# One-core attention and expert kernel: the sinks' rows of v loaded once and split on GpSimd, buffers cleared by VectorE, the first weights' rounding moved

## What is computed

```python
def _attn_ref(q, k, v, n_sink, window):       # q, k, v: 2 x 8 x 768 x 64, n_sink 4, window 128
    scores = scale * np.matmul(q, k.transpose(0, 1, 3, 2))
    keep = is_sink | in_window                # the first 4 keys, and the last 128 up to the query
    scores = np.where(keep, scores, -1e9)
    a = np.exp(scores - np.max(scores, axis=-1, keepdims=True))
    a = a / (np.sum(a, axis=-1, keepdims=True) + 1e-09)
    return np.matmul(a, v)

x = attention, laid out as 1536 tokens x 512
x = layernorm(h * softmax(h)) * g_ln @ w_out       # h = x @ w_in, 512 -> 1024 -> 512
out = sum over 8 experts of P[:, e] * (relu(x @ w1[e]) @ w2[e])   # P: Sinkhorn gate of x @ w_gate
```

## Time and profile before

| | |
|---|---|
| median of 3 runs | 1252.02 us (1251.76 to 1252.05) |
| the profiled execution, its own time | 1253.09 us |
| its span, first to last instruction | 1251.3 us |
| TensorE's granted clock | 1.00 over the whole span |
| busy: PE, DVE, ACT, POOL | 99%, 55%, 29%, 43% |
| DMA engines busy, mean, slices of 31 us | 6, 4 and 4 tenths in the first three, then 0 to 1 |

### The profile page before, as it was taken

The page is one execution under the profiler, slowest core; times in us unless marked ns, Lnnn a source line. Parts: engine busy times, 40 slices in busy tenths (PEclk is TensorE's granted clock), DMA queues, the critical chain, the costliest instruction groups (busy, mean ns, idle before and its releaser), DMA issues.

```text
span 1251.3 us, 18785 instructions
## 1 busy us (share of the span) xinstructions
PE 1236.2 (99%) x6446; PEld 1097.3 (88%) x6446; DVE 691.7 (55%) x1348; ACT 365.1 (29%) x832; POOL 535.7 (43%) x625
## 2 busy tenths in 40 slices
PE   7999999999999999999999999999999999999998
PEld 4558899989988999999999999999999999999997
DVE  7895734356665555555555555555555555555554
ACT  7884634312233222222222222222222222222221
POOL 7772315644444444444444444444444444444440
PEclk9999999999999999999999999999999999999999
DMA  6440000111110111111111111111111111111102
GB/s 204 156 149 18 1 1 1 34 35 34 34 35 28 38 36 36 34 34 34 34 34 34 34 34 34 34 34 34 34 34 34 34 34 34 34 34 34 35 18 101
DMA packets 57264, 53.13 MB, mean 42 GB/s; under 512 B 4352, under 2 KB 44544, under 8 KB 57216
## 3 DMA queue, kind: packets, MB, share of 16 engines
q1 hardware_dynamic: 56928, 52.19, 13.1%
q10 hardware_dynamic: 288, 0.33, 0.1%
HBM read 49.35 MB, written 3.15 MB: 42 GB/s over the span
## 4 chain that ended last, share of the span: by engine, by line
PE 95%; ACT 2%; DVE 2%; DMA 1%; issue 1%; SPq 0%; DVEq 0%; ACTq 0%
PE ps L797 30%; PE ps L798 30%; PE ps L799 30%; PE ps L722 2%; PE ps L766 1%; PE ps L742 1%; PE ps L847 1%; ACT probs L1042 1%; ACT acc L1218 1%; DVE probs L1270 1%; DMA k_sb<-kT 0%; PE ps L977 0%; DVE xw L1303 0%; ACT xw L1066 0%; DMA q_sb<-qT 0%
## 5 line engine op out<-in xcount | busy, mean ns | idle before, releaser
L1528 DVE SCALAR_TENSOR_TENSOR acc<-ps,gate_now,acc 128x512 f32<-128x512 f32 x336 | 252.1, 750 | 166.2 <-PE ps L799 162.0
L797 PE MATMUL ps<-ring 128*128 128x512 f32 x768 | 300.6, 391 | 0.0
L798 PE MATMUL ps<-ring 128*128 128x512 f32 x768 | 299.8, 390 | 0.0
L799 PE MATMUL ps<-ring 128*128 128x512 f32 x768 | 299.2, 390 | 0.0
L1200 ACT ACTIVATE sums<-ps 128x384 f32<-128x384 f32 x192 | 94.4, 492 | 597.8 <-PE ps L799 597.8
L1504 DVE TENSOR_TENSOR sums<-ps,sums 128x384 f32<-128x384 f32 x192 | 106.9, 557 | 158.2 <-ACT sums L1200 106.9
L799 PEld LDWEIGHTS ps<-ring 128*128 128x128 f32 x768 | 144.3, 188 | 30.9
L797 PEld LDWEIGHTS ps<-ring 128*128 128x128 f32 x768 | 144.2, 188 | 27.9 <-DVE acc L1524 0.4
L798 PEld LDWEIGHTS ps<-ring 128*128 128x128 f32 x768 | 144.2, 188 | 25.8
L642 POOL TENSOR_TENSOR w_raw<-w_raw 128x256 f32<-128x256 f32 x32 | 23.7, 741 | 321.3 <-PE ps L799 321.3
L797 PE MATMUL ps<-xw,ring 128*128 128x384 f32 x448 | 152.5, 340 | 0.3 <-ACT sums L1200 0.2
(11 more groups left out here) (148 smaller groups left out, 1765.2 us busy)
## 6 DMA issues: line engine op xcount, KB each, us to landing
w_in<-w_exp SPq DMA_DIRECT2D x64, 256.0 KB, 3.2
w_raw<-w_exp SPq DMA_DIRECT2D x64, 128.0 KB, 2.8
w_raw<-w_exp SPq DMA_DIRECT2D x32, 256.0 KB, 3.2
v_sb<-v SPq DMA_DIRECT2D x16, 192.0 KB
out<-acc SPq DMA_DIRECT2D x12, 256.0 KB, 2.0
q_sb<-qT SPq DMA_DIRECT2D x7, 384.0 KB, 4.4
k_sb<-kT SPq DMA_DIRECT2D x7, 384.0 KB, 4.9
k_sb<-kT SPq DMA_DIRECT2D x9, 256.0 KB, 5.7
```

The lines of the kernel that those rows point to most:

```text
L797: pe.matmul(o, ws[0], xs[0], start=first, stop=False, skip_group_check=True)
L798: pe.matmul(o, ws[0], xs[1], start=False, stop=False, skip_group_check=True)
L799: return pe.matmul(o, ws[1], xs[0], start=False, stop=last, skip_group_check=True)
L1528: dve.scalar_tensor_tensor(out=acc[:, T, :], in0=y_bank(u, T), scalar=gate_now[:, T:T + 1], in1=acc[:, T, :], op0=ALU.mult, op1=ALU.add).t ...
```

## The change

The sinks' rows of v get a tile for all 8 pairs (`[72, 8, 128]` in place of `[72, 2, 128]`) and are loaded once, by six DMAs, which stand behind the first segment in SP's queue. POOL rounds them and takes the rest, for two pairs at a time, behind pairs 0, 2, 4 and 6 (`split_v_sinks`); `rest_v_sinks` on DVE is gone. The memsets of `v_sink`, `sink_cols`, `wg` and `ones` go from POOL to DVE, ahead of its first work. In pair 0 POOL rounds segment 0 between `normalise` 0 and `normalise` 1, takes the rest of `w_in` behind `lay_sinks`, and the rest of `w_out` behind `split_sinks`.

```diff
-        v_sink = sb("v_sink", [SINK_ROWS, 2, P], F32, in_a)
-        v_sink_r = sb("v_sink_r", [SINK_ROWS, 2, P], F32R, in_a)
+        v_sink = sb("v_sink", [SINK_ROWS, PAIRS, P], F32, in_a)
+        v_sink_r = sb("v_sink_r", [SINK_ROWS, PAIRS, P], F32R, in_a)
...
             def load_v(p, h):
                 sp.dma_start(v_sb[:, p % 2, h, :], v[p, h]).then_inc(v_loaded[p % 2], 16)
+
+            def load_v_sinks(h):
                 for row in (0, 32, 64):
                     row += h * NS
-                    sp.dma_start(v_sink[row:row + NS, p % 2, h * DH:(h + 1) * DH],
-                                 v[p, h, 0:NS, 0:DH]).then_inc(v_loaded[p % 2], 16)
+                    sp.dma_start(v_sink[row:row + NS, :, h * DH:(h + 1) * DH],
+                                 v[:, h, 0:NS, 0:DH].rearrange("p n d -> n p d")).then_inc(v_sinks_loaded, 16)
...
-            sp.wait_ge(consts, 2)
             for h in range(2):
                 load_v(0, h)
             load_segments(0)
+            sp.wait_ge(v_sinks_clear, 1)
+            for h in range(2):
+                load_v_sinks(h)
...
-            pool.memset(v_sink[:, :], 0.0).then_inc(consts, 1)
...
-            pool.memset(sink_cols[:, :, :].bitcast(F32), 0.0).then_inc(sinks_hi, 1)
...
-            pool.memset(ones[:, :], 1.0).then_inc(consts, 1)
-            pool.memset(wg[:, :, :].bitcast(F32), 0.0).then_inc(consts, 1)
...
+            def split_v_sinks(p):
+
+                two = slice(p, p + 2)
                 if p == 0:
-                    pool.wait_ge(consts, 2)
-                pool.tensor_scalar(v_sink_r[:, p % 2, :], v_sink[:, p % 2, :], 1.0, 0.0,
+                    pool.wait_ge(v_sinks_loaded, 96)
+                pool.tensor_scalar(v_sink_r[:, two, :], v_sink[:, two, :], 1.0, 0.0,
                                    ALU.mult, ALU.add).then_inc(v_sinks_hi, 1)
+                pool.wait_ge(v_sinks_hi, p // 2 + 1)
+                low = v_sink_r[64:SINK_ROWS, two, :]
+                pool.tensor_tensor(low, v_sink[64:SINK_ROWS, two, :], low.bitcast(F32),
+                                   ALU.subtract).then_inc(v_sinks_split, 1)
+                pool.wait_ge(v_sinks_split, p // 2 + 1)
...
             for p in range(PAIRS):
                 normalise(p, 0)
-                if p > 0:
+                if p == 0:
+                    round_segments(0)
+                else:
                     rest_w_in(p)
                 normalise(p, 1)
                 if p + 1 < PAIRS:
                     lay_sinks(p + 1)
                 if p == 0:
-                    round_segments(0)
                     rest_w_in(0)
-                rest_w_out(p)
+                else:
+                    rest_w_out(p)
                 if p == 4:
                     rest_router()
                 normalise(p, 2)
                 split_sinks(p)
-                round_v_sinks(p)
+                if p == 0:
+                    rest_w_out(0)
+                if p % 2 == 0:
+                    split_v_sinks(p)
                 if p + 1 < PAIRS:
                     round_segments(p + 1)
...
-                if t == 3 and p > 0:
-                    rest_v_sinks(p - 1)
...
+            dve.memset(v_sink[:, :, :], 0.0).then_inc(v_sinks_clear, 1)
+            dve.memset(sink_cols[:, :, :].bitcast(F32), 0.0).then_inc(sink_cols_clear, 1)
+            dve.memset(wg[:, :, :].bitcast(F32), 0.0).then_inc(router_clear, 1)
+            dve.memset(ones[:, :], 1.0).then_inc(ones_set, 1)
             dve.memset(top[:, 3:4], -0.5).then_inc(exponent, 1)
```

More of the change, by code:

```diff
@@ L219, in solu_moe @@
         sinks_hi, sinks_split = sem("sinks_hi"), sem("sinks_split")
+        sink_cols_clear, router_clear, ones_set = sem("sink_cols_clear"), sem("router_clear"), sem("ones_set")
+        v_sinks_clear, v_sinks_loaded = sem("v_sinks_clear"), sem("v_sinks_loaded")
         v_sinks_hi, v_sinks_split = sem("v_sinks_hi"), sem("v_sinks_split")
@@ L503, in _ @@
             pool.memset(mask1[:, 0:NS], 0.0).then_inc(masks, 1)
-            pool.memset(sink_cols[:, :, :].bitcast(F32), 0.0).then_inc(sinks_hi, 1)
-            pool.wait_ge(consts, 2)
+            pool.wait_ge(consts, 1)
             pool.affine_select(out=ident[:, :], in_=ident[:, :], compare_op=ALU.not_equal, fill=1.0,
                                base=0, pattern=[[-1, P]], channel_multiplier=1).then_inc(consts, 1)
-            pool.memset(ones[:, :], 1.0).then_inc(consts, 1)
-            pool.memset(wg[:, :, :].bitcast(F32), 0.0).then_inc(consts, 1)
             def normalise(p, b):
@@ L534, in split_sinks @@
                     pool.wait_ge(probs_ready[h], BATCHES * (p + 1))
-                if p > 0:
+                if p == 0:
+                    pool.wait_ge(sink_cols_clear, 1)
+                else:
                     pool.wait_ge(pT_full, T_USES * (p - 1) + SINK_USE + 1)
@@ L541, in split_sinks @@
                 last.then_inc(sinks_hi, 1)
-                pool.wait_ge(sinks_hi, p + 2)
+                pool.wait_ge(sinks_hi, p + 1)
                 pool.tensor_tensor(sink_cols[:, :, 32:32 + n], a, sink_cols[:, :, 0:n].bitcast(F32),
@@ L758, in pv @@
                 if b == 0:
-                    pe.wait_ge(v_loaded[p % 2], 128 * (p // 2 + 1))
+                    pe.wait_ge(v_loaded[p % 2], 32 * (p // 2 + 1))
                     if p > 0:
@@ L771, in pv_sinks @@
                 pe.wait_ge(*copied(p, SINK_USE))
-                pe.wait_ge(v_sinks_split, p + 1)
-                pe.matmul(x_psum(2, QT), v_sink_r[:, p % 2, :], sinkT[:, :],
+                pe.wait_ge(v_sinks_split, p // 2 + 1)
+                pe.matmul(x_psum(2, QT), v_sink_r[:, p, :], sinkT[:, :],
                           start=False, stop=True, skip_group_check=True).then_inc(x_full, 1)
@@ L788, in back @@
                     if p == 0:
-                        pe.wait_ge(consts, 3)
+                        pe.wait_ge(consts, 2)
                     turn(p, 0)
@@ L990, in gate_step @@
                 if step == "logits":
+                    pe.wait_ge(ones_set, 1)
                     gate_logits()
@@ L1091, in _ @@
                     act.wait_ge(small_loaded, 32)
-                    act.wait_ge(consts, 5)
+                    act.wait_ge(router_clear, 1)
                     act.activation(wg[:, :, WG_AT:WG_AT + EXPERTS], wg_raw[:, :, :], ACT.Copy).then_inc(wg_ready, 1)
@@ L1292, in copy_pT @@
                                 t_bank(p, use)[:, 0:(n1 - n0) * P]).then_inc(pT_dve, 1)
[L1294 to L1298, removed]
             def rest_x(p):
@@ L1403, in _ @@
             copy_pT(PAIRS - 1, 2, 1)
-            rest_v_sinks(PAIRS - 1)
             solu(1)
```

## The result

| | before | changed |
|---|---|---|
| median of 9 runs each | 1252.48 us (1251.76 to 1253.64) | 1255.12 us (1254.02 to 1257.06) |
| the profiled execution, its own time | 1253.09 us | 1257.06 us |
| its span | 1251.3 us | 1255.3 us |

The ratio is 1.0021, with an interval of 1.0011 to 1.0031: the changed kernel is longer by 2.6 us, about the 0.2% that a measurement here can tell. The profiled execution was the longest of its nine, so its trace shows more of the loss (+4.0 us of span) than the median does.

The account below looks back on a forecast made before the run. TensorE was taken to bound the kernel (95% of the chain), everything from 94 us on moving as a block. A later k, +3.0, and removed rests, -1.4, gave +1.6 us on 1252.02: 1253.6 us, range 1251.2 to 1255.5.

Parts of the forecast that it names:

- Segment 0's landing: Pair 0's first loads: landings unchanged at 11.2 and 11.9 us although issued over 2 us earlier, DMA engines being full.
- The rival of an early landing: Segment 0 lands at 8.9 us, L579 ends about 16.9, 1.4 us later than before; total 1251.6 us; chance 0.10.
- GpSimd's first pair: POOL's new order in pair 0: it waits for data, second normalise near 12.5, L579 ends at 18.8, 3.4 us later.
- k of pair 2: Load before pair 2's scores, issued behind the segment that awaits L579: lands at 26.6 instead of 23.67, 3.0 us later.
- The removed rests: L1297 gone from VectorE: shorter ScalarE waits in pairs 2 to 6, gain 1.4 us (0.9 to 1.9).
- loss of half in pairs 3 and 5: POOL's later work meets VectorE's small instructions in pairs 3 and 5: 0.37 of their 0.74 us gain lost.
- ScalarE's idle time: ScalarE's waits for the maxima of t = 5 in pairs 2 to 6, the most each can gain: 1.77 us together.
- the gain is not passed on: Rival: pairs 3 and 5 lose their gain, other gaps open ahead of ScalarE elsewhere; 1255.4 us; chance 0.20.
- the one that has all of L1297's time count: Rival: each L1297 worth its full time, some 4.5 us over seven pairs; 1249.3 us with early landing; chance 0.07.
- Memsets: Four memsets on VectorE at the start: 2.2 us, ended by 3.1, before its first work at 3.96; price nothing.
- the step that let only the stall that ends last count: Before pair 2: pair 1's normalise 0 ends about 24, ahead of k, so only the stall on k is priced.

Follow-up runs that it names:

- the second profile: The changed kernel run again, unaltered, as base of three follow-ups: 1256.53 us, ratio 1.0027 to the kernel before.
- old order with and without the instruction: Changed kernel with GpSimd's old order of pair 0; with v's rests back on VectorE 1252.40 us, ratio 0.9996; without, 1250.33 us, ratio 0.9978.
- the filled stall: Changed kernel with 17 extra identity matmuls where TensorE waits, 12 before pair 1's later transposes, 5 before k: 1254.15 us, ratio 1.0011.
- the move alone: Kernel before with only GpSimd's new order in pair 0: 1257.22 us, ratio 1.0032; two runs at mean clock 1.00, six at 0.996 or 0.997.
- old order: Changed kernel with GpSimd's order of pair 0 as before, all else kept: 1250.33 us, ratio 0.9978; repeated, 1250.39 us, 0.9979.
- q and k first: q and k of pair 2 issued ahead of segment 1: on the changed kernel 1253.58 us, ratio 1.0007; with GpSimd's old order too, 1250.33 us, 0.9975.

## Why the prediction came out as it did

The time forecast was 1253.6 us, in a range of 1251.2 to 1255.5; the median is 1255.12, near its upper end. The ratio, 1.0021, lies on the line between "the same" and "slower". Step by step:

- **Segment 0's landing.** Right: 11.8 for `w_in` and 12.5 for `w_out`, against 11.2 and 11.9, although `w_in` is issued at 4.98 in place of 7.2. The load of `w_in` took 6.80 us in place of 4.0, while the DMA engines' share from 3 to 11 us was 1.05. In the four other profiles with the early rounding and the early issue it took 5.6 to 7.1 us. The rival of an early landing, with its 4.0 us, falls. (Its own sum is 0.3 us off: 13.2 + 2.17 + 1.27 is 16.6, not 16.9, which changes nothing.)
- **GpSimd's first pair.** Right in its order and its waits. The second `normalise` starts at 13.12 (forecast 12.5) and L579 ends at 19.36 (18.8), both later by what the landing was later.
- **k of pair 2.** Forecast 26.6, landed 26.25 (26.69 in the second profile): +2.6 us, where the sum had +3.0. From L579's end to the landing it is 6.89 us, under the forecast 7.2 to 8.5: k's last load took 4.88 us, where rows 8 had 5.2 to 6.5.
- **The removed rests.** Forecast -1.4, at most -1.77; measured -1.9 (old order with and without the instruction), and the mechanism is the one named. Two sizes were off. No loss of half in pairs 3 and 5 shows: all four periods are 11.05 or 11.06 us, and each of pairs 3 to 6 gained 0.30 to 0.33 us. And pair 2 gained 0.67 us, over the 0.43 of ScalarE's idle time that was taken for the most. The rival "the gain is not passed on" falls, and so does the one that has all of L1297's time count: 0.31 a period against a median duration of 0.50.
- **Memsets.** Right. VectorE's timeline has them from 1.01 to 3.32, 2.19 us in all for 2336 elements a partition, and the first maximum at 5.09 (4.96 before):

```profile
1.01 0.91 DVE L1330 MEMSET v_sink<- 72x1024 f32 x1 [1.01 <-PEq L1606]
1.93 0.30 DVE L1331 MEMSET sink_cols<- 128x288 f32 x1
2.37 0.81 DVE L1332 MEMSET wg<- 128x896 f32 x1
3.15 0.17 DVE L1333 MEMSET ones<- 128x128 f32 x1
```

  The estimate of 2.4 us, from the page of the Trainium skill that the prediction names (VectorE: DVE Perf Modes, "Zero memsets can be issued as uint32 (trn2)"), is near: the trace has 0.89 ns an element for the largest of the four.

- **What failed: the step that let only the stall that ends last count.** The prediction worked out that `normalise` 0 of pair 1 would end at about 24 (24.31 in the trace), "still ahead of k", and gave that no price. But TensorE ran dry for it, 2.96 us, before it waited for k. The end of the stall was forecast well; what TensorE did in it was not asked. It stood for 4.34 us with only 0.55 us of work between, and its clock fell at 25.6, inside the second of the two waits. That is +3.6 us in the profiled execution, and by the filled stall and the two groups of the move alone 2.4 to 3.2 us. No term and no bound of the sum had it. The missed +2.4 to 3.6 was partly made up by a stall 0.4 smaller and a gain 0.5 greater. That the time still fell into the range is luck: its upper bound stands for a lost gain, and the gain was not lost. Of the 1.5 us by which the median lies above the forecast, 0.46 are the kernel before, whose median was 1252.02 in three runs and 1252.48 in nine.

The Trainium skill (TensorE: Matmul & The Clock Gate, "Part 1: The HAM clock gate") has the throttled state as the default, from which activity releases the array. The trace agrees in kind: 0.50 behind the waits, 1.00 again after some 10 us at the lower level, most of them work. By that rule a sum of stalls needs TensorE's idleness as a second question beside their end.

**What stays open.** In the traces the clock fell in the wait that followed one of 2.96 us, behind a wait of 2.08 us (before the next of 1.10), and within one of 3.02 us; it stayed full through waits of 1.35 and 1.07 us and of 0.61 and 1.01 us. With one profile of each kernel this is no threshold, and runs of one kernel differ in it: 5 of the 87 runs of the kernel before have a low mean clock as well. How much of the difference between runs comes from the clock of the start, and how much from the landings, isn't settled either. And the gain of 1.9 us is shown in the old order only: in the new one (changed against the move alone, 1256.53 against 1257.22) the two differ by 0.7 us, with intervals of more than a microsecond on each.

## What to carry to other kernels

When an instruction that waits for a DMA is moved up in an engine's list, what counts is what is queued behind it: here the move cost 4.4 us by itself, and the same change without it is 2.5 us faster than before. For each stall that grows ask two things, when it ends and how long TensorE has nothing to do in it: here the lower clock cost 2.4 to 3.6 us on top of a stall that had grown by 2.6. And measure the parts of a mixed change apart: this one held -2.5 and +4.4 to +6.2 us, and its sum looked like a small loss.

## What was not expected of the hardware

- With waits of 2.96 and 1.38 us TensorE's granted clock was 0.50 from 25.6, inside the second, to 35.8 us, though it was busy for 8.70 of the 9 us from 26 on. With q and k first it was 0.50 from 22.8 to 29.7, and fell 1.8 us into a wait.
- At the start the clock column doesn't show the level. In the profile with the old order and q and k first it reads 1.00 throughout, while eight transposes take 1.97 us at 15.16 and 1.09 at 20.64. The Trainium skill (TensorE: Matmul & The Clock Gate, "Seeing it yourself") warns that the records of the clock can be unreliable on trn2. The trace bears it out, and the duration of a repeated matmul is the surer sign here.
- The full clock of the start came, by such durations, between 8.4 and 20.3 us in the twelve profiles of kernels that begin with the same matmuls.
- Issuing a load 2.2 us earlier into full DMA engines (share 1.05 from 3 to 11 us) brought it in no earlier in the profile of the changed kernel: 6.80 us to landing in place of 4.0.
